# A folding stage that sums in split precision: column-pair sums as three float32r products, differences in float32

## What is computed

```python
h_filt = (np.maximum(pos_emb @ w1, 0.0) @ w2) * np.exp(-0.01 * pos)[:, None]
u = x * v                                   # x, v: 2 x 12480 x 128
L = 2 * S
y = np.fft.irfft(np.fft.rfft(u, n=L, axis=1) * np.fft.rfft(h_filt, n=L, axis=0)[None], n=L, axis=1)[:, :S, :]
attn = x * y
h = attn.reshape(B * S, D) @ w_in           # d_ff = 2048
P = a[0] + a[1] * h + a[2] * h**2 + a[3] * h**3
Q = 1.0 + abs(b[0]) * abs(h) + abs(b[1]) * h**2
out = (P / (Q + 1e-6)) @ w_out
```

## Time and profile before

| | us |
|---|---|
| median of three runs | 2047.46 |
| lowest, highest | 2046.43, 2047.89 |
| profiled execution, its own time | 2047.94 |
| its span (first to last instruction) | 2046.2 |
| PE busy over the span | 1940.0 (95%) |
| DVE, POOL, ACT busy | 1761.0, 1685.2, 1655.4 |
| last `plus_copy` or `minus_copy` of the first stage | 257.4 |

### The profile page before, as it was taken

One profiled execution on the slowest core, in us unless ns is written; L12 is line 12 of the kernel. 1 busy time (PEld: TensorE's weight loads), 2 busy tenths in 40 slices (PEclk: granted clock), 3 DMA queues, 4 the chain that ended last, 5 costly groups with the idle time before them and its releaser, 6 DMA issues. The chain is left out here.

```text
span 2046.2 us, 27063 instructions
## 1 busy us (share of the span) xinstructions
PE 1940.0 (95%) x7956; PEld 1301.0 (64%) x7956; DVE 1761.0 (86%) x2375; ACT 1655.4 (81%) x2454; POOL 1685.2 (82%) x1126
## 2 busy tenths in 40 slices
PE   6999959999789999999999999999999999999997
PEld 3454537777656666666666666666666666666664
DVE  3565449999869999999999999999999999999997
ACT  1333325555569999999999999999999999999998
POOL 3665514444369999999999999999999999999997
PEclk9999979999979999999999999999999999999999
DMA  6888698999721111111111111111111111111100
GB/s 167 278 284 278 212 233 218 240 245 245 188 51 33 33 33 33 33 33 33 37 33 33 33 36 44 46 33 33 33 33 33 33 33 33 33 33 33 36 10 13
DMA packets 69066, 181.79 MB, mean 89 GB/s; under 512 B 4937, under 2 KB 11490, under 8 KB 66034
## 3 DMA queue, kind: packets, MB, share of 16 engines
q1 hardware_dynamic: 68922, 180.09, 32.1%
HBM read 108.31 MB, written 71.76 MB: 88 GB/s over the span
## 5 line engine op out<-in xcount | busy, mean ns | idle before, releaser
L701 POOL TENSOR_TENSOR den<-slope,mag 128x832 f32<-128x832 f32 x480 | 949.1, 1977 | 0.0
L937 PE MATMUL acc_p<-g_s,w_out_k 128*128 128x416 f32 x1920 | 767.1, 522 | 43.8 <-DVE g_s L854 23.2
L821 DVE SCALAR_TENSOR_TENSOR num<-square,level,h_p 128x832 f32<-128x832 f32 x480 | 517.9, 1079 | 82.7 <-ACT square L732 41.1
L693 POOL TENSOR_SCALAR slope<-mag,den_c 128x832 f32<-128x832 f32 x480 | 500.8, 1043 | 63.5 <-DVE mag L816 46.2
L854 DVE SCALAR_TENSOR_TENSOR g_s<-num,ratio,r_p 128x832 f32<-128x832 f32 x480 | 517.9, 1079 | 12.4 <-ACT r_p L748 4.6
L937 PEld LDWEIGHTS acc_p<-g_s,w_out_k 128*128 128x128 f32 x1920 | 341.3, 189 | 290.3 <-issue 183.7
L732 ACT ACTIVATE square<-h_p,centre 128x832 f32<-128x832 f32 x480 | 469.5, 978 | 36.5 <-DVE mag L816 32.8
L926 PE MATMUL h_p<-xy_hi,w_lo 128*128 128x416 f32 x960 | 457.0, 476 | 5.3 <-DVE num L821 2.8
L741 ACT ACTIVATE den<-den 128x832 f32<-128x832 f32 x480 | 442.1, 921 | 1.7 <-POOL den L701 1.5
L748 ACT ACTIVATE r_p<-den 128x832 f32<-128x832 f32 x480 | 427.8, 891 | 0.9 <-DVE g_s L854 0.7
L926 PE MATMUL h_p<-xy_lo,w_hi 128*128 128x416 f32 x960 | 338.1, 352 | 0.0
(11 more groups left out here) (72 smaller groups left out, 2111.9 us busy)
## 6 DMA issues: line engine op xcount, KB each, us to landing
bent<-bent_s SPq DMA_DIRECT2D x30, 1152.0 KB, 6.8
bin_s<-bent SPq DMA_DIRECT2D x23, 1440.0 KB, 10.6
x_s<-in_x SPq DMA_DIRECT2D x59, 416.0 KB
vin_s<-back SPq DMA_DIRECT2D x29, 768.0 KB, 5.9
back<-back_s SPq DMA_DIRECT2D x23, 960.0 KB, 11.6
v_s<-in_v SPq DMA_DIRECT2D x30, 416.0 KB
out<-o_s SPq DMA_DIRECT2D x60, 208.0 KB
merged_s<-table_merged SPq DMA_DIRECT2D x24, 225.0 KB, 3.6
```

What stands on the lines that cost most here:

```text
L693: nc.gpsimd.tensor_scalar(slope[:, q % DEEP], mag[:, q % DEEP], den_c[:, 1:2], den_c[:, 0:1], ALU.mult, ALU.add).then_inc(slope_done, 1)
L701: nc.gpsimd.tensor_tensor(den[:, q % DEEP], slope[:, q % DEEP], mag[:, q % DEEP], ALU.mult).then_inc(den_done, 1)
L821: nc.vector.scalar_tensor_tensor(out=num[:, q % NUMS], in0=square[:, q % SQUARES], scalar=level[:], in1=h_p[:, q % 2, :, 0:TOK], op0=ALU.a ...
L937: mm = nc.tensor.matmul(acc_p[:, 0:TOK], w_out_k[:, ft], g_s[:, q % DEEP, t], start=(ft == 0), stop=(ft == FT - 1))
```

## The change

The sum tile `plus` is split as `plus_hi` (float32r copy, made by ACT in the new `high`) and `plus_lo` (the rest, subtracted by POOL in the new `low`), half a block at a time. So is the part of `fold` that the plus side uses: `fold_hi` by ACT and `fold_lo` by DVE, once, before anything else on these engines, and PE waits for both before its first instruction. A plus pair on PE becomes two groups of three float32r products in place of two float32 ones; a minus pair stays as it is. PE's plus folds wait for `plus_lo_done`. `high` for block `b+1` is put on ACT behind `posT_copy` of either half (`LEAD_SPLIT` = 1; the constant `LEAD_SUMS`, which nothing used, goes). `high` waits for the first of the half's two sums and for the fold of the block that held its slot. POOL's list gets `low` behind each pair of sums. The four tiles `w_in_s`, `w_out_s`, `w_hi` and `w_lo` are allocated after the first stage's tiles are given back, in front of the second stage; what loads and uses them is unchanged.

```diff
@@ gpsimd
+                def low(b, half):
+                    s, at = b % SLOTS, slice(half * HALF, (half + 1) * HALF)
+                    pool.wait_ge(plus_hi_done, b * 2 + half + 1)
+                    nc.gpsimd.tensor_tensor(plus_lo[:, s, at], plus[:, s, at], plus_hi[:, s, at].bitcast(F32),
+                                            ALU.subtract).then_inc(plus_lo_done, 1)
+
                 for b in range(FOLDS):
                     for half in range(2):
                         sums(b, half)
+                        low(b, half)
@@ scalar
+                def high(b, half):
+                    s, at = b % SLOTS, slice(half * HALF, (half + 1) * HALF)
+                    act.wait_ge(sums_done, b * 4 + half * 2 + 1)
+                    if b >= SLOTS:
+                        act.wait_ge(g_done, (b - SLOTS + 1) * JB * 2)
+                    nc.scalar.activation(plus_hi[:, s, at], plus[:, s, at], ACT.Copy).then_inc(plus_hi_done, 1)
+
                 act.wait_ge(consts_in, CONSTS)
+                nc.scalar.activation(fold_hi[:], fold[:, 0:2 * K1], ACT.Copy).then_inc(fold_split, 1)
                 for b in range(-LEAD_MAKE, FOLDS):
                     make, now = inside(b + LEAD_MAKE), inside(b)
+                    split = inside(b + LEAD_SPLIT)
                     if make:
                         posT_copy(b + LEAD_MAKE, 0)
+                    if split:
+                        high(b + LEAD_SPLIT, 0)
                     if now:
                         plus_copy(b, 0)
...
                     if make:
                         posT_copy(b + LEAD_MAKE, 1)
+                    if split:
+                        high(b + LEAD_SPLIT, 1)
                     if now:
                         plus_copy(b, 2)
@@ vector
+                dve.wait_ge(fold_split, 1)
+                nc.vector.tensor_tensor(fold_lo[:], fold[:, 0:2 * K1], fold_hi[:].bitcast(F32), ALU.subtract).then_inc(fold_split, 1)
@@ tensor
-                    pe.wait_ge(sums_done, b * 4 + i // HALF * 2 + side + 1)
+                    if side == 0:
+                        pe.wait_ge(plus_lo_done, b * 2 + i // HALF + 1)
+                    else:
+                        pe.wait_ge(sums_done, b * 4 + i // HALF * 2 + 2)
                     if unit >= RING:
                         pe.wait_ge((plus_out, minus_out)[(unit - RING) % 2], (unit - RING) // 2 + 1)
-                    f = (plus, minus)[side]
                     for c in range(2):
-                        w = fold[:, (side + c) * K1:(side + c + 1) * K1]
-                        mm = nc.tensor.matmul(g_p[0:K1, unit % RING, c, 0:COLS], w, f[:, s, i, :], start=True, stop=True)
+                        to, at = g_p[0:K1, unit % RING, c, 0:COLS], slice((side + c) * K1, (side + c + 1) * K1)
+                        if side == 0:
+                            for term, (w, f) in enumerate(((fold_lo, plus_hi), (fold_hi, plus_hi), (fold_hi, plus_lo))):
+                                mm = nc.tensor.matmul(to, w[:, at], f[:, s, i, :], start=(term == 0), stop=(term == 2))
+                        else:
+                            mm = nc.tensor.matmul(to, fold[:, at], minus[:, s, i, :], start=True, stop=True)
                     mm.then_inc(g_done, 1)
 
                 pe.wait_ge(consts_in, CONSTS)
+                pe.wait_ge(fold_split, 2)
```

More of the change, by code:

```diff
@@ L107, in hyena_mlp @@
         turn_j = kept("turn_j", [J, K1, 3])
-        w_in_s, w_out_s = kept("w_in_s", [D, FF]), kept("w_out_s", [128, FT, D])
-        w_hi, w_lo = kept("w_hi", [D, FF], F32R), kept("w_lo", [D, FF], F32R)
         coef = kept("coef", [128, 4])
@@ L123, in hyena_mlp @@
             fold = sb("fold", [ROWS, 3 * K1])
+            fold_hi, fold_lo = sb("fold_hi", [ROWS, 2 * K1], F32R), sb("fold_lo", [ROWS, 2 * K1], F32R)
             window = sb("window", [FILTER_ROWS, SIDES, HALF_J])
@@ L133, in hyena_mlp @@
             plus, minus = sb("plus", [ROWS, SLOTS, JB, COLS]), sb("minus", [ROWS, SLOTS, JB, COLS])
+            plus_hi, plus_lo = sb("plus_hi", [ROWS, SLOTS, JB, COLS], F32R), sb("plus_lo", [ROWS, SLOTS, JB, COLS], F32R)
             bent_s = sb("bent_s", [K1, SLOTS, 2, JB, 2, COLS])
@@ L142, in hyena_mlp @@
             pad_zero, prod_done, filt_done, sums_done = sem("pad_zero"), sem("prod_done"), sem("filt_done"), sem("sums_done")
+            plus_hi_done, plus_lo_done, fold_split = sem("plus_hi_done"), sem("plus_lo_done"), sem("fold_split")
             posT_ps, posT_sb, hid_ps, hid_sb, filt_ps = (sem(n) for n in ("posT_ps", "posT_sb", "hid_ps", "hid_sb", "filt_ps"))
@@ L147, in hyena_mlp @@
             HALF = JB // 2
-            LEAD_LOAD, LEAD_MAKE, LEAD_SUMS = 4, 2, 1
+            LEAD_LOAD, LEAD_MAKE, LEAD_SPLIT = 4, 2, 1
             def inside(b):
@@ L396, in _ @@
                         fold_pair(b, 3, 1)
+        w_in_s, w_out_s = kept("w_in_s", [D, FF]), kept("w_out_s", [128, FT, D])
+        w_hi, w_lo = kept("w_hi", [D, FF], F32R), kept("w_lo", [D, FF], F32R)
         with ExitStack() as ctx:
```

## The result

The changed kernel takes 2093.64 us in the median of four runs (2091.76 to 2094.91), against 2047.68 before. The ratio is 1.0221, with a 95% interval of 1.0209 to 1.0233: 2.2% slower. The forecast was 2062.6, in a range up to 2076. The sign was right and the size wrong by a factor of three. The profiled execution took 2094.07, its span is 2092.3. The last `bent_s` copy of the first stage ends at 301.9 us instead of 257.4, so 44.5 of the 46.1 us between the two profiled executions lie in that stage.

The account below looks back on a forecast made before the run. The prediction took PE's instruction order to bound the first stage; +16.2 us (wait for POOL's sum), -2.1 (last blocks) and +1.0 (start) on 2047.94 gave 2063.0, hence a median of 2062.6 us, range 2047 to 2076.

Parts of the forecast that it names:

- PE sets the pace, and a wait in its way is paid in full: First stage: PE's instruction order bounds it, PE never waits now, and any added wait costs its full length.
- Part 1: PE's plus pair: six float32r matmuls take 1.03 us against 1.29, a gain of 0.26 per pair, 1.04 per block.
- Part 2: ACT's plus_hi copy waits for POOL's long first sum; PE stands still 2.39 us, net +1.35 per block, +16.2 in all.
- Part 3: POOL's two subtractions per block, 1.81 us each (up to 2.37), don't bound; the second half hides with 0.5 us spare.
- Parts 4 and 5: Last two first-stage blocks: -2.1 us; start: +1.0 us (bounds -1 and +5); later stages: zero, 1.5 either side.
- rival D: PE's six products get no cheaper at 1.29 us: 60 pairs lose 0.26 each, time 2078 us; no separate chance.
- the bounds of 0.6 to 2.1 us per block: First stage, main case (chance 0.76): net loss per block from bounds on copy, pair and low; 2053 to 2074 us.
- rival C: PE's 2.4 us stalls halve its clock, costing at least 2 us in each of 12 blocks: 2086 and more; chance 0.04.
- Rival A: POOL's first sum takes 1.81 us instead of 3.62, PE stands still 0.58, kernel gets faster: 2040.9 us; chance 0.12.

## Why the prediction was wrong

**PE sets the pace, and a wait in its way is paid in full**: right; with PE's list free of waits the stage took 14.21 us per block, with one wait of 2.2 us and a full clock 16.47.

**Part 1, the products**: 1.03 us for six. They start 0.17 to 0.18 apart in the trace, so the step is right, but behind another kind of matmul the first step takes 0.24. Per pair the gain is 0.24 where the waits are the same, against 0.26 forecast.

**Part 2, the order on ACT**: right to about a tenth. Copy 0.84 as taken; `filter_rows` 5.59 us behind the start of POOL's sum, forecast 5.69 (135.52 - 129.83); PE's idleness 2.2, forecast 2.39. Without the falls of the clock a block is 1.31 longer, forecast 1.35, and the kernel with the filler takes 2060.5 us, which is the forecast of 2062.6 less 2. That it is so near has some luck in it: the stall cost 16.47 - 14.21 = 2.26 where 2.39 was forecast and the products saved 0.95 where 1.04 was, and the two misses cancel.

**Part 3, POOL**: `plus_lo` takes 1.80, and PE waited 0.9 us in all for it. The second half had no wait, as said. What I called half a microsecond to spare was not there in a shorter block, as the run with one half moved shows.

**Parts 4 and 5**: the last blocks saved 0.7 where I took 2.1: from the first sum of 1.8 us to the stage's last copy it is 301.9 - 281.2 = 20.7 us, before 257.4 - 236.0 = 21.4, and PE waits 0.8 us there for ACT's `bent_s`. The first steady sum starts at 54.49 instead of 54.01, so the start cost 0.5 where I took 1.0. The later stages took 1790.4 us in this profile and 1788.8 before; the forecast was zero.

**Sums that were off without mattering**: rival D counts 60 pairs, but one pair of each of the 12 blocks lies ahead of the wait and changes nothing, so 48 count and its time is 2075; the run with float32 folds and the filler took 2071.6. And the bounds of 0.6 to 2.1 us per block don't follow from the parts named with them, which give 1.35 - 0.21 - 0.21 = 0.93 and 1.35 + 0.11 + 0.27 = 1.73, or 2.3 with a late `low`.

**What failed** is rival C, which I gave 0.04 and should have made a term of the sum: "PE's stall of 2.4 us each block makes its clock fall to half". It was priced at 2 us per block at least and cost 2.50, in twelve blocks; the stage ended at 301.9 where 272 was forecast, which is nearly all of the 31 us that were missing. The step behind that chance was the inference from the earlier trace rows: one wait of 2.60 us ahead of 282.53 with a full clock was taken to show that a wait of 2.4 is harmless. It was a single case in another stage, and the other side had only been seen at 4 us. In this stage the clock fell behind 12 of 12 waits of 2.2 us and behind 11 of 12 of 1.6, and behind none of those up to 0.9. Nor was the other stage safe: there 2.63 us at that very place had a fall behind it in one run.

The Trainium skill (TensorE: Matmul & The Clock Gate, HAM oscillation — how this bites in real kernels) describes a loop in which short bursts of matmuls start at the low clock after each wait for a DMA. The trace agrees on the repetition: the clock was at half for 0.12 x 2 = 24% of the 256 us. It differs in two things: the waits on that page are 3 to 5 us long and those here 2.2, and the clock here was still full when PE took up its work.

**Rival A** stays refuted in its cause: the sum took 3.6 us in 12 of 12 blocks. Where it did take 1.83, in the run with the product moved, the time was 2054.0 and not A's 2040.9, since the operation of 3.82 us behind it brought the second half a wait of 0.88. The Trainium skill (SBUF — State Buffer, Who interferes with whom) says that a DVE instruction with two SBUF inputs contends with a GpSimd one that reads SBUF, and that the order of issue decides who waits. The first half holds in these traces. The second can't be judged by the start of the product: POOL's operation started 0.74 us ahead of it and ended long behind it. The order that goes with the outcome in all runs is that of POOL's start and the start of the copy ahead of the product. Whether the product counts as issued from there on, no trace shows; if it does, the rule holds too.

## What to carry to other kernels

Before a copy is put into an in-order engine's list, look at what stands behind it: here a copy of 0.84 us on an idle engine, which itself had to wait for GpSimd, became 2.2 us of waiting on the busiest, and moving it two places down turned 2.2% slower into 0.65% faster. A wait on TensorE has a second price where its clock falls behind it, and here that was larger than the wait's own (2.50 us per block against 2.26); filler matmuls into a free bank are a cheap way to measure it by itself. And a slack found in one schedule doesn't hold in a faster one: check it again with the new block time.

## What the runs showed of the hardware

In the first stage, waits of TensorE of 2.2 us were each followed by a stretch at 0.50, single ones too, and the stretches behind waits cost 2.50 us per block (18.97 against 16.47). Waits of 1.6 us did it in 11 of 12 blocks, those of 0.26, 0.42, 0.49, 0.81 and 0.88 never. The length of the wait is not the whole of it: in the second stage waits of 2.60 and 2.29 us had no fall behind them and one of 2.63 had. What tells them apart stays open; no run was made for it.

A GpSimd operation of 1.8 us that starts 0.14 us into a VectorE copy with a product of two SBUF tiles queued behind it takes 3.6 to 3.8 us, whether it is a first sum or a `plus_lo`. If it starts 0.19 us ahead of that copy, it takes 1.81, and the product takes 1.83 instead of 1.21.
